# Attention and two expert stages on one core: the second expert's weights loaded after routing, tile stores moved to SP, q and k fetched two pairs ahead, first value means by matmul

## The chip, the cores and the metric

The kernel runs on one core of a Trainium2 chip (trn2). The metric is the device time of one execution in microseconds (us), lower is better. The inputs are float32 and the output is float32.

## What is computed

```python
# attention: B=2, H=8, S=768, D=64, block 32, window 16
k_sum = k.reshape(B, H, nb, block, D).max(axis=3)
v_sum = v.reshape(B, H, nb, block, D).mean(axis=3)
scores_l = scale * q @ k.T          # kept where |i-j| < 16, else -1e9
scores_s = scale * q @ k_sum.T + log(block)
a = softmax(concat(scores_l, scores_s))
x = a @ concat(v, v_sum)            # 1536 tokens of 512

# first expert stage: N=1536, 8 experts, D=512, F=1024, top 2
noisy = x @ w_gate + log1p(exp(x @ w_noise)) * noise
for e in range(E):                  # each token goes to its top two experts
    out[mask] += top2_w * (relu(x[mask] @ w1[e]) @ w2[e])

# second stage, dense: F=2048
h = x @ w_in; g = maximum(0.01 * h, h); out = g @ w_out
```

Every product with weights is made of three products of split numbers: a float32 is split into a part `hi` that TensorE takes in one pass and the rest `lo`, and hi·hi, lo·hi and hi·lo are added up in PSUM.

## The kernel before, in words

Each engine has its program in its own order, written out by hand; semaphores are all that ties them.

**Attention.** The 16 heads go in 8 pairs (`PAIRS`), a pair's 12 units of 64 rows in 3 groups (`GROUPS`), so there are 24 steps c. Per pair PE turns q (`turn_q`, L1044) and k (`turn_k`, L1053) by transposes, and per step it makes the scores (`score`, L1066), turns the probabilities (`turn_probs`, L1075) and weighs the values (`weigh`, L1090). Between them lie DVE's maximum and normalisation and ACT's exp and copies. PE's program for pair n is score(3n), turn_probs, turn_k(n+1), weigh, score(3n+1), ..., score(3n+2), turn_probs, turn_q(n+2), weigh(3n). Tokens of finished pairs are also turned and multiplied with the gate weights (L1103, L1112).

SP issues the loads and stores of this stage, in one queue: q and k of a pair (`load_q`, `load_k`), the windows of v for a pair (`load_windows`, three DMAs), the block means of v spread over the units (`load_means`), and the finished tokens (`store_x`). Rows of q, k and v are 256 bytes long and lie apart in the target, so a pair costs 2·2·768 = 3072 packets for q and k, 24·64 + 2·16·23 = 2272 for the windows, 2·24·12 = 576 for the means and 768 for the tokens, 6688 in all. There is one buffer `qk_nat` for q and k: q of pair n+1 is fetched once q of pair n has been turned. The block means come from POOL: `block_means(i)` (L465) halves 128 blocks of 32 rows six times, SP stores the result in HBM and reads it back; there are three such parts, and the first pair needs the first of them.

POOL then splits the weights of expert 0 and, from the fifth turned k on, of expert 1 (`load_weights`): 8 chunks of 512 KB, each a DMA (L476), `w_hi` (L495) and `w_lo` (L497), 4 staging buffers. `w1_ready` is raised after chunk 4, `w2_ready` after chunk 8. The split weights have two places (`par` 0 and 1), so expert e takes the place of e-2.

**Routing.** DVE, ACT and PE pick each token's experts, ending with `token_of` (L925), the token of every row of every tile. There are 31 tiles of 128 rows.

**First expert stage.** POOL gathers the tokens of each tile by indirect DMA: tiles 0 to 2 into `x_first` (L548), tiles 3 and up into a ring of 7 places `x_ring` (L538), from which POOL stores them tile by tile in HBM (`store_tile`, L529, 4 tiles behind the gather). A place is gathered into again once its store has landed. Tiles 3 to 23 are gathered in one go before the weights of expert 2, tiles 24 and 25 after them, 26 to 30 after those of expert 3.

SP reads a tile back into one of two places `x_row` (`load_row`, L373) and stores the tile's result from the single buffer `y_row` (`store_row`, L377): load_row(3), load_row(4), store_row(0), the filling of spare rows (L392), load_row(5), store_row(1), and so on. PE's program for tile t (`tile`, from L1223) is: turn x of t (L1177), second product of tile t-2 (hT and w2), turn h of t-1 (L1182), first product of t (L1190 for both products). Before the second product of t-2 PE waits here:

```python
                pe.wait_ge(w2_ready, loads)
                pe.wait_ge(hT_lo_ready, t + 1)
                if not first:
                    pe.wait_ge(y_ready, t)
```

and DVE does, per tile t of its loop, `xT_out(t)`, `y_out(t - 2)`, `hT_out(t - 1)`, where y_out copies the product out of PSUM:

```python
                if not first:
                    dve.wait_ge(y_stored, 16 * t)
                nc.vector.tensor_copy(y_row[:], bank).then_inc(y_ready, 1)
```

**Second stage.** Rows are picked by indirect DMA and PE makes the two dense products (L1274 to L1276, L1289 to L1291). The change doesn't touch it.

## Time and profile before

| | us |
|---|---|
| three runs | 831.04, 832.78, 834.69 |
| median | 832.78 |
| the profiled execution, its own time | 829.91 |
| its span | 828.3 |
| PE busy | 754.7 (91%) |
| POOL busy | 392.5 (47%) |
| DVE busy | 272.5 (33%) |
| ACT busy | 224.1 (27%) |

The span is the time from the first to the last instruction of the trace; the execution's own time is 1.6 us longer. By stages, in us from the span's start: attention until 130, routing until 153, the first expert stage until 545, the second to the end. Times below are positions in this one execution. "PE L1044 <- DMA qk_nat" in a table of waits reads: PE stood idle before the instruction of line 1044, and the DMA into qk_nat was what ended the wait.

### The profile page before, as it was taken

How to read it: one execution, taken by the hardware profiler on the slowest of the kernel's cores; microseconds unless marked ns; L12 is line 12 of the kernel's file. 1: busy time of each engine (PE TensorE's matmuls, PEld its weight loads, DVE VectorE, ACT ScalarE, POOL GpSimd, SP SyncE). 2: the span in 40 equal slices, each digit the busy share in tenths (PEclk: the TensorE clock that was granted, in tenths of full speed). 3: DMA queues.
4: the chain of work that ended last, by engine and by line, in shares of the span. 5: the costliest groups of instructions: out<-in, count | busy, mean ns of one | idle time of the engine just before them, and what ended most of it. 6: DMA issues, size and time to landing. Idle time of an engine off the chain costs nothing.

```text
span 828.3 us, 12304 instructions
## 1 busy us (share of the span) xinstructions
PE 754.7 (91%) x4026; PEld 632.2 (76%) x4027; DVE 272.5 (33%) x521; ACT 224.1 (27%) x405; POOL 392.5 (47%) x350
## 2 busy tenths in 40 slices
PE   3569892699999999999999999979999999999997
PEld 3458782578878888888888888878788887888885
DVE  3456556321221221222222122136343324432223
ACT  2557562022112212112112121225222222222221
POOL 5687860465786967888788783610011001000000
PEclk9889895599999999999999999989999999999999
DMA  9799970389726364353444441334011101010001
GB/s 213 177 286 227 268 128 13 112 288 297 242 89 215 127 214 173 120 187 143 144 142 156 138 141 38 114 127 154 13 39 51 51 1 50 0 51 0 0 1 51
DMA packets 87422, 103.15 MB, mean 125 GB/s; under 512 B 55680, under 2 KB 61824, under 8 KB 86976
## 3 DMA queue, kind: packets, MB, share of 16 engines
q0 software_dynamic: 17008, 59.52, 22.0%
q1 hardware_dynamic: 69328, 43.22, 20.5%
q8 instruction: 17, 0.28, 0.2%
q10 hardware_dynamic: 1056, 0.03, 0.1%
q14 instruction: 13, 0.11, 0.0%
HBM read 80.89 MB, written 23.69 MB: 126 GB/s over the span
## 4 chain that ended last, share of the span: by engine, by line
PE 61%; POOL 13%; DMA 10%; SPq 7%; DVE 4%; issue 4%; ACT 1%; POOLq 0%; DVEq 0%
PE p L1190 23%; POOL w_lo L497 6%; PE p L1274 5%; PE p L1276 5%; PE p L1275 5%; PE p L1289 5%; PE p L1291 5%; PE p L1290 5%; DMA x_by_tile<-x_ring 3%; POOL w_hi L495 3%; SPq L294 2%; DMA x_ring<-x_tokens,token_of 2%; POOL x_ring L538 2%; PE p L1182 2%; DMA stage<-in_moe_w 2%
## 5 line engine op out<-in xcount | busy, mean ns | idle before, releaser
L497 POOL TENSOR_TENSOR w_lo<-stage,w_hi 128x1024 fp32r<-128x1024 f32 x72 | 171.8, 2386 | 6.0
L1190 PE MATMUL p<-w_hi,xT_hi 128*128 x248 | 100.1, 404 | 3.3 <-DVE xT_lo L929 1.6
L584 POOL DMA_INDIRECT y_pick<-y_by_tile,slots x20 | 19.1, 955 | 165.9 <-PE p L1261 150.2
L1190 PE MATMUL p<-w_lo,xT_hi 128*128 x248 | 97.2, 392 | 0.0
L1190 PE MATMUL p<-w_hi,xT_lo 128*128 x248 | 97.2, 392 | 0.0
L1190 PE MATMUL p<-w_hi,hT_hi 128*128 x240 | 96.5, 402 | 0.0
L1190 PE MATMUL p<-w_lo,hT_hi 128*128 x240 | 93.9, 391 | 0.0
L1190 PE MATMUL p<-w_hi,hT_lo 128*128 x240 | 93.5, 390 | 0.0
L495 POOL TENSOR_SCALAR w_hi<-stage 128x1024 fp32r<-128x1024 f32 x72 | 75.9, 1054 | 18.9 <-DMA stage<-in_moe_w 14.8
L1274 PE MATMUL p<-f_xT_hi,w_hi 128*128 (+2 forms) x200 | 78.3, 392 | 1.3 <-DVE f_xT_lo L978 1.3
L1275 PE MATMUL p<-f_xT_lo,w_hi 128*128 (+2 forms) x200 | 77.2, 386 | 0.0
L1276 PE MATMUL p<-f_xT_hi,w_lo 128*128 (+2 forms) x200 | 77.1, 386 | 0.0
L1289 PE MATMUL p<-w_hi,f_hT_hi 128*128 128x512 f32 x192 | 75.0, 390 | 1.4 <-DVE f_hT_lo L988 1.3
L1291 PE MATMUL p<-w_hi,f_hT_lo 128*128 128x512 f32 x192 | 74.7, 389 | 0.0
L1290 PE MATMUL p<-w_lo,f_hT_hi 128*128 128x512 f32 x192 | 74.7, 389 | 0.0
L686 ACT CAST hT_hi<-p 128x1024 fp32r<-128x1024 f32 x30 | 30.5, 1015 | 156.5 <-PE p L1182 143.3
L929 DVE TENSOR_TENSOR xT_lo<-p,xT_hi 128x512 fp32r<-128x512 f32 x31 | 21.4, 692 | 154.6 <-ACT xT_hi L683 149.9
L986 DVE SCALAR_TENSOR_TENSOR f_h<-p,f_h 128x512 f32<-128x512 f32 x48 | 33.2, 691 | 116.6 <-ACT f_h L708 116.6
L681 ACT ACTIVATE h_row<-p 128x1024 f32<-128x1024 f32 x30 | 30.8, 1027 | 139.7 <-PE p L1190 134.6
L708 ACT COPY f_h<-p 128x512 f32<-128x512 f32 x48 | 28.2, 588 | 142.2 <-PE p L1276 142.2
L935 DVE COPY y_row<-p 128x512 f32<-128x512 f32 x31 | 21.5, 693 | 115.6 <-PE p L1190 115.6
L476 POOL DMA_DIRECT2D stage<-in_moe_w x64 | 41.5, 650 | 33.0 <-POOL w_lo L497 22.5
(184 smaller groups left out, 1253.8 us busy)
## 6 DMA issues: line engine op xcount, KB each, us to landing
stage<-in_moe_w POOLq DMA_DIRECT2D x64, 512.0 KB, 4.9
y_by_tile<-y_row SPq DMA_DIRECT2D x31, 256.0 KB
x_by_tile<-x_ring POOLq DMA_DIRECT2D x28, 256.0 KB, 6.9
x_row<-x_by_tile SPq DMA_DIRECT2D x28, 256.0 KB
qk_nat<-in_q SPq DMA_DIRECT2D x16, 192.0 KB, 5.6
qk_nat<-in_k SPq DMA_DIRECT2D x16, 192.0 KB, 4.7
stage<-in_v SPq DMA_DIRECT2D x3, 1024.0 KB, 7.8
v_win<-in_v SPq DMA_DIRECT2D x8, 384.0 KB
```

The costliest lines, as they stand in the source:

```text
L476: pool.dma_start(stage_view(c % STAGES, c), source(c)).then_inc(staged[c % STAGES], 16)
L495: pool.tensor_scalar(w_hi[:, par, cols], stage[:, c % STAGES, :], 1.0, 1.0, ALU.mult, ALU.mult).then_inc(hi_split, 1)
L497: pool.tensor_tensor(w_lo[:, par, cols], stage[:, c % STAGES, :], w_hi[:, par, cols].bitcast(F32), ALU.subtract).then_inc(lo_split, 1)
L681: nc.scalar.activation(h_row[:], h_bank[:], ACT.Relu).then_inc(h_ready, 1)
L986: nc.vector.scalar_tensor_tensor(out=h, in0=f_h_bank[c % 2], scalar=0.01, in1=h, op0=ALU.mult, op1=ALU.max).then_inc(f_leaky_done, 1)
L1190: last = nc.tensor.matmul(bank, a, w, start=(c == 0 and i == 0), stop=(c == left_hi.shape[1] - 1 and i == 2))
L1274: nc.tensor.matmul(to, hi, f_xT_hi[:, cols], start=(k == 0), stop=False)
L1275: nc.tensor.matmul(to, hi, f_xT_lo[:, cols], start=False, stop=False)
L1276: last = nc.tensor.matmul(to, lo, f_xT_hi[:, cols], start=False, stop=(k == KD - 1))
L1289: nc.tensor.matmul(f_y_bank[m], f_hT_hi[:, c % 2, rows], hi, start=(c == 0), stop=False)
L1290: nc.tensor.matmul(f_y_bank[m], f_hT_hi[:, c % 2, rows], lo, start=False, stop=False)
L1291: last = nc.tensor.matmul(f_y_bank[m], f_hT_lo[:, c % 2, rows], hi, start=False, stop=(c == FC - 1))
```

## The change

Six things move, and the line numbers of the changed kernel are up to 30 higher.

1. q and k have two buffers each (`qk_nat` and `qk_other`, which lies in the second place of w_hi) and are fetched up to two pairs ahead.
2. POOL loads expert 1 no longer during attention. Three of its chunks are fetched before `token_of`; the splitting stands after the gathers of tiles 3 to 9, and the gathers of tiles 10 to 23 stand between its chunks 4 and 5 (`between`).
3. `store_tile` goes from POOL to SP. SP's program is now: stores of tiles 3 to 9, load_row(3), load_row(4), stores of tiles 10 to 23, store_row(0), and from there as before.
4. The first pair's block means are made by PE: 12 small matmuls of the windows with `in_block` (1/32 where a row is in a block), one PSUM bank, one ACT copy. The three parts of `block_means` cover the other 14 heads, the last with 80 blocks, and are stored one by one inside SP's loop of pairs: each of the last two with a wait for its landing.
5. PE's first score comes before turn_q(1) and turn_k(1) comes later, with the same moves on ACT and DVE.
6. POOL builds `in_block` (four instructions) before the masks.

```diff
+MEAN_ROWS = [(2 * NB, 2 * NB + P), (2 * NB + P, 2 * NB + 2 * P), (2 * NB + 2 * P, B * H * NB)]
...
-LAG = 4
...
+        with ExitStack() as room:
+            sb("first_w_hi", [P, WCOLS], where=room)
+            qk_other = sb("qk_other", [P, 2, TPB, 2, D], where=room)
+            v_mean = sb("v_mean", [P, 3, D], where=room)
+            in_block = sb("in_block", [WK, 2 * NB - 2], where=room)
...
-            qk_nat = sb("qk_nat", [P, 2, TPB, 2, D], where=room)
+            qk_nat = [sb("qk_nat", [P, 2, TPB, 2, D], where=room), qk_other]
...
-            v_mean = xT_gate[:, 0:3 * D].rearrange("p (i d) -> p i d", i=3)
...
         def _(sp):
             def load_q(n):
                 for h in range(2):
-                    sp.dma_start(qk_nat[:, 0, :, h, :], q_pairs[2 * n + h]).then_inc(q_loaded, 16)
+                    sp.dma_start(qk_nat[n % 2][:, 0, :, h, :], q_pairs[2 * n + h]).then_inc(q_loaded[n % 2], 16)
...
             def load_rows(i):
 
-                sp.dma_start(stage[:, 2 * (i % 2):2 * (i % 2) + 2, :].rearrange("p a n -> p (a n)"),
-                             v_rows[i * P:(i + 1) * P, :]).then_inc(v_nat_loaded[i], 16)
+                first, end = MEAN_ROWS[i]
+                sp.dma_start(stage[0:end - first, 2 * (i % 2):2 * (i % 2) + 2, :].rearrange("p a n -> p (a n)"),
+                             v_rows[first:end, :]).then_inc(v_nat_loaded[i], 16)
...
@@ -320,42 +327,39 @@
 
             load_q(0)
             load_k(0)
-            load_rows(0)
             sp.wait_ge(consts_done, 2)
             load_windows(0)
+            load_q(1)
+            load_k(1)
+            load_rows(0)
+            load_windows(1)
             sp.wait_ge(q_turned, 1)
-            load_q(1)
+            load_q(2)
             sp.wait_ge(k_turned, 1)
-            load_k(1)
+            load_k(2)
+            store_means(0)
             load_rows(1)
-            sp.wait_ge(q_turned, 2)
-            load_q(2)
-            load_windows(1)
-            store_means(0)
-            load_rows(2)
             sp.wait_ge(v_mean_stored[0], 16)
-            load_means(0)
             load_means(1)
             for n in range(PAIRS):
-                if n + 2 < PAIRS:
+                if n + 3 < PAIRS:
+                    sp.wait_ge(q_turned, n + 2)
+                    load_q(n + 3)
                     sp.wait_ge(k_turned, n + 2)
-                    load_k(n + 2)
+                    load_k(n + 3)
+                if n == 0:
+                    load_rows(2)
                 if n >= 1:
                     store_x(n - 1, 0)
                     if n + 1 < PAIRS:
                         sp.wait_ge(weighed, GROUPS * n)
                         load_windows(n + 1)
+                        if n < 3:
+                            store_means(n)
+                            sp.wait_ge(v_mean_stored[n], 16)
                         load_means(n + 1)
                     store_x(n - 1, 1)
                     store_x(n - 1, 2)
-                if n + 3 < PAIRS:
-                    sp.wait_ge(q_turned, n + 3)
-                    load_q(n + 3)
-                if n == 0:
-                    for i in (1, 2):
-                        store_means(i)
-                    for i in (1, 2):
-                        sp.wait_ge(v_mean_stored[i], 16)
...
-            def load_row(t, r, uses):
-
-                sp.wait_ge(xs_stored[r], 16 * uses)
+            def load_row(t):
+
+                sp.wait_ge(xs_stored[(t - FIRST) % RING], 16 * ((t - FIRST) // RING + 1))
                 half = (t - FIRST) % ROWS
-                sp.dma_start(x_row[:, half, :], xs_dram[bass.ds(t * P, P), :]).then_inc(x_row_loaded[half], 16)
+                sp.dma_start(x_row[:, half, :], xs_dram[t * P:(t + 1) * P, :]).then_inc(x_row_loaded[half], 16)
 
             def store_row(t):
                 sp.wait_ge(y_ready, t + 1)
                 sp.dma_start(ys_dram[bass.ds(t * P, P), :], y_row[:]).then_inc(y_stored, 16)
 
-            def turn_over(t):
-
+            def store_tile(t):
                 r, uses = (t - FIRST) % RING, (t - FIRST) // RING + 1
-                if t >= FIRST + ROWS:
-                    sp.wait_ge(x_turned, t - ROWS + 1)
-                load_row(t, r, uses)
-                if t >= FIRST + 1:
-                    store_row(t - FIRST - 1)
-
-            assert (TILES - FIRST) % RING == 0
-            for t in range(FIRST, TILES):
-                turn_over(t)
-                if t == FIRST + 1:
+                sp.wait_ge(gathered[r], 16 * uses)
+                sp.dma_start(xs_dram[t * P:(t + 1) * P, :], x_ring[:, r, :]).then_inc(xs_stored[r], 16)
+
+            for t in range(FIRST, FIRST + RING):
+                store_tile(t)
+            for t in range(FIRST, FIRST + ROWS):
+                load_row(t)
+            for t in range(FIRST + RING, 2 * NT):
+                store_tile(t)
+            store_row(0)
+            for t in range(FIRST + ROWS, TILES):
+                if t >= 2 * NT:
+                    store_tile(t)
+                sp.wait_ge(x_turned, t - ROWS + 1)
+                load_row(t)
+                store_row(t - FIRST - 1)
+                if t == FIRST + ROWS:
                     sp.dma_start(ys_dram[FULL * P:TILES * P, :], x_dram[0:(TILES - FULL) * P, :]).then_inc(spare_filled, 16)
...
+
+            link(pool.memset(in_block[:], 0.0))
+            blocks = in_block[:, NB - 2:NB]
+            link(pool.memset(blocks, 1.0 / BLOCK))
+            link(pool.affine_select(out=blocks, in_=blocks, compare_op=ALU.is_ge, fill=0.0, base=-WINDOW, pattern=[[-BLOCK, 2]], channel_multiplier=1))
+            signal(pool.affine_select(out=blocks, in_=blocks, compare_op=ALU.is_ge, fill=0.0, base=WINDOW + BLOCK - 1, pattern=[[BLOCK, 2]], channel_multiplier=-1))
...
+            def fetch(source, c):
+                pool.dma_start(stage_view(c % STAGES, c), source(c)).then_inc(staged[c % STAGES], 16)
+
+            def load_weights(source, e, par, reused=True, fetched=False, between=None):
+
+                for c in range(0 if fetched else STAGES - 1):
+                    fetch(source, c)
...
+                    if c == KD and between:
+                        between()
...
             load_weights(lambda c: weight_piece(0, c), 0, 0, reused=False)
-            pool.wait_ge(k_turned, 5)
-            load_weights(lambda c: weight_piece(1, c), 1, 1, reused=False)
...
+            for c in range(STAGES - 1):
+                fetch(lambda c: weight_piece(1, c), c)
             pool.wait_ge(token_of_done, 1)
...
-            def store_tile(t):
-                r, uses = ring_slot(t)
-                pool.wait_ge(gathered[r], 16 * uses)
-                pool.dma_start(xs_dram[t * P:(t + 1) * P, :], x_ring[:, r, :]).then_inc(xs_stored[r], 16)
...
                         pool.wait_ge(xs_stored[r], 16 * (uses - 1))
                     pool.indirect_dma_start(out=x_ring[:, r, :], out_offset=None, in_=x_dram,
                                             in_offset=bass.IndirectOffsetOnAxis(ap=token_of[:, t:t + 1], axis=0)).then_inc(gathered[r], 16)
-                    if t - LAG >= first:
-                        store_tile(t - LAG)
-                for t in range(max(first, end - LAG), end):
-                    store_tile(t)
...
-            gather_tiles(FIRST, 2 * NT)
+            gather_tiles(FIRST, FIRST + RING)
+            load_weights(lambda c: weight_piece(1, c), 1, 1, reused=False, fetched=True, between=lambda: gather_tiles(FIRST + RING, 2 * NT))
...
-            q_part(1)
             for n in range(PAIRS):
                 c = GROUPS * n
                 if c >= 1:
                     probs_out(c - 1)
                 softmax_exp(c)
-                if n + 1 < PAIRS:
+                if n == 0:
+                    act.wait_ge(first_means_done, 1)
+                    nc.scalar.copy(v_win[WK:KC, 0, :, :, 0:D], first_mean_bank.rearrange("x (h d) -> x h d", h=2).unsqueeze(2).to_broadcast([NB, 2, UNITS, D])).then_inc(first_means_ready, 1)
+                    q_part(1)
+                elif n + 1 < PAIRS:
                     k_part(n + 1)
 
                 probs_out(c)
                 softmax_exp(c + 1)
+                if n == 0:
+                    k_part(1)
                 if n >= 2:
-                    if n == 2:
-                        for i in range(3):
-                            act.wait_ge(v_mean_stored[i], 16)
...
-            q_part(1)
-            dve.wait_ge(consts_done, 3)
+            dve.wait_ge(consts_done, 4)
             for n in range(PAIRS):
                 for g in range(GROUPS):
                     c = GROUPS * n + g
                     if c >= 3:
                         normalise(c - 3)
                     softmax_max(c)
-                    if g == 1 and n + 1 < PAIRS:
+                    if c == 0:
+                        q_part(1)
+                    if c == 2:
+                        k_blocks(1)
+                    if g == 1 and 1 <= n < PAIRS - 1:
                         k_blocks(n + 1)
                     if g == 2 and n + 2 < PAIRS:
...
-                if g == 0:
-                    pe.wait_ge(v_loaded[n % 2], 80 * (n // 2 + 1))
+                if c == 0:
+                    pe.wait_ge(first_means_ready, 1)
+                if g == 0 and n >= 1:
+                    pe.wait_ge(v_loaded[n % 2], (80 if n % 2 else 48) + 80 * (n // 2))
...
+            def first_means():
+
+                pe.wait_ge(v_loaded[0], 48)
+                pe.wait_ge(consts_done, 3)
+                for u in range(UNITS):
+                    last = nc.tensor.matmul(first_mean_bank, in_block[:, NB - 2 - 2 * u:2 * NB - 2 - 2 * u], v_win[0:WK, 0, :, u, 0:D],
+                                            start=(u == 0), stop=(u == UNITS - 1))
+                last.then_inc(first_means_done, 1)
...
-            turn_q(1)
             for n in range(PAIRS):
                 c = GROUPS * n
                 score(c)
                 if c >= 1:
                     turn_probs(c - 1)
-                if n + 1 < PAIRS:
+                if n == 0:
+                    first_means()
+                    turn_q(1)
+                elif n + 1 < PAIRS:
                     turn_k(n + 1)
                 if c >= 2:
                     weigh(c - 2)
 
                 score(c + 1)
                 turn_probs(c)
+                if n == 0:
+                    turn_k(1)
                 if n >= 2:
                     gate_turn(n - 2)
```

SP around the first expert stage; x_by_tile is the tiles' place in HBM, y_by_tile the results'. Before:

```order
L318 DMA x_tokens<-x_out 128x2x128 x3
L373 DMA x_row<-x_by_tile 128x512 x2
L377 DMA y_by_tile<-y_row 128x512
L392 DMA y_by_tile<-x_tokens 32x14336
L373 DMA x_row<-x_by_tile 128x512
L377 DMA y_by_tile<-y_row 128x512
```

and in the change:

```order
L325 DMA x_tokens<-x_out 128x2x128 x3
L386 DMA x_by_tile<-x_ring 128x512 x7
L377 DMA x_row<-x_by_tile 128x512 x2
L386 DMA x_by_tile<-x_ring 128x512 x14
L381 DMA y_by_tile<-y_row 128x512
L377 DMA x_row<-x_by_tile 128x512
L381 DMA y_by_tile<-y_row 128x512
L402 DMA y_by_tile<-x_tokens 32x14336
```

Twenty-one stores of tiles now stand in SP's program, fourteen of them ahead of the first store of a result.

POOL after routing, before:

```order
L548 DMA x_first<-x_tokens,token_of 128x512 x3
L538 DMA x_ring<-x_tokens,token_of 128x512 x5
L529 DMA x_by_tile<-x_ring 128x512
L538 DMA x_ring<-x_tokens,token_of 128x512
...
L529 DMA x_by_tile<-x_ring 128x512 x5
L476 DMA stage<-in_moe_w 128x1024 x3
```

and in the change:

```order
L557 DMA x_first<-x_tokens,token_of 128x512 x3
L553 DMA x_ring<-x_tokens,token_of 128x512 x7
L491 DMA stage<-in_moe_w 128x1024
L515 TENSOR_SCALAR w_hi<-stage 128x1024
L517 TENSOR_TENSOR w_lo<-stage,w_hi 128x1024
...
L491 DMA stage<-in_moe_w 128x2x512
L553 DMA x_ring<-x_tokens,token_of 128x512 x14
L515 TENSOR_SCALAR w_hi<-stage 128x1024
L517 TENSOR_TENSOR w_lo<-stage,w_hi 128x1024
```

The gathers of tiles 10 to 23 (x14) have four chunks of weights ahead of them and the other four behind.

SP in attention in the change, the second pair's turn of the loop:

```order
L286 DMA qk_nat<-in_q 128x6x64 x2
L290 DMA qk_nat<-in_k 128x6x64 x2
L325 DMA x_tokens<-x_out 128x2x128
L298 DMA v_win<-in_v 64x24x64
L299 DMA v_win<-in_v 16x23x64
L300 DMA v_win<-in_v 16x23x64
L318 DMA v_means<-v_mean 128x64
L307 DMA v_win<-v_means 24x12x64 x2
L325 DMA x_tokens<-x_out 128x2x128 x2
```

q and k stand at its head, for three pairs on, and the store of a part of the means stands with its wait between the windows and the reading of the means.

## Rows read from the trace of the kernel before

**Rows 1.** Windows: start:end length, busy us PE, PEld, DVE, ACT, POOL, PEclk, DMA share, GB/s
```profile
36.00:40.00 4.00, 4.00 (x54) 3.52 (x53) 2.85 (x7) 3.42 (x7) 3.13 (x7) 0.98 0.25 42
76.00:104.00 28.00, 22.96 (x225) 20.42 (x224) 15.83 (x36) 17.04 (x41) 21.50 (x18) 0.88 1.18 273
300.00:400.00 100.00, 99.65 (x487) 82.85 (x486) 21.57 (x25) 20.49 (x25) 78.30 (x63) 1.00 0.49 172
```
**Rows 2.** Waits of PE from 40 to 116: us in total, times, longest
```profile
PE p L1044 <- DMA qk_nat<-in_q: 9.6, 3, 5.4
PE p L1053 <- DMA qk_nat<-in_k: 3.0, 2, 2.1
```
**Rows 3.** Waits from 0 to 40
```profile
PE p L1090 <- DMA v_win<-v_means: 6.3, 1, 6.3
```
**Rows 4.** DMA queues from 76 to 104 (q1 SP's, q0 POOL's): packets, MB, share
```profile
q1 hardware_dynamic: 12839, 3.59, 74.9%
q0 software_dynamic: 1091, 4.01, 42.4%
```
**Rows 5.** DMA queues from 111 to 116
```profile
q1 hardware_dynamic: 2560, 0.81, 123.0%
```
**Rows 6.** Timeline of PE in attention: start, us, what [idle before, releaser]
```profile
33.54 2.06 PE L1066 MATMUL p<-kT,q_diag 128*128 128x120 f32 x8
...
58.58 1.54 PE L1044 MATMUL p<-ident,qk_nat 128*128 128x128 f32 x6 [5.44 <-DMA qk_nat<-in_q]
...
71.12 0.88 PE L1044 MATMUL p<-ident,qk_nat 128*128 128x128 f32 x6
```
**Rows 7.** Timeline of POOL: gathers of tiles 3, 4 and 23
```profile
157.00 0.95 POOL L538 DMA_INDIRECT x_ring<-x_tokens,token_of  x1 [0.30 <-issue]
158.25 0.94 POOL L538 DMA_INDIRECT x_ring<-x_tokens,token_of  x1 [0.30 <-issue]
...
200.77 0.97 POOL L538 DMA_INDIRECT x_ring<-x_tokens,token_of  x1 [0.30 <-DMA x_by_tile<-x_ring]
```
**Rows 8.** Timeline of POOL: chunk 1's w_hi and chunk 4's w_lo of expert 2
```profile
213.18 1.06 POOL L495 TENSOR_SCALAR w_hi<-stage 128x1024 fp32r<-128x1024 f32 x1 [2.05 <-DMA stage<-in_moe_w]
...
229.09 2.37 POOL L497 TENSOR_TENSOR w_lo<-stage,w_hi 128x1024 fp32r<-128x1024 f32 x1
```
**Rows 9.** Timeline of PE: first products of tiles 0 and 6, tile 2's second product
```profile
159.26 0.79 PE L1190 MATMUL p<-w_hi,xT_hi 128*128 x1 [1.60 <-DVE xT_lo L929]
...
162.69 0.40 PE L1190 MATMUL p<-w_lo,xT_hi 128*128 x1
...
199.48 0.48 PE L1190 MATMUL p<-w_hi,hT_hi 128*128 x1
...
231.74 0.49 PE L1190 MATMUL p<-w_hi,xT_hi 128*128 x1 [1.00 <-POOLq L500]
```
**Rows 10.** Timeline of DVE: tile 1's result, tile 2's hT_lo
```profile
193.09 0.69 DVE L935 COPY y_row<-p 128x512 f32<-128x512 f32 x1 [3.81 <-PE p L1190]
194.91 1.22 DVE L929 TENSOR_TENSOR hT_lo<-p,hT_hi 128x1024 fp32r<-128x1024 f32 x1 [1.13 <-ACT hT_hi L686]
```
**Rows 11.** Timeline of SP: store of tile 0's result
```profile
181.44 0.32 SPq L377 DMA_DIRECT2D y_by_tile<-y_row  x1
```
**Rows 12.** DMA queues from 157 to 208
```profile
q0 software_dynamic: 3306, 10.83, 66.6%
q1 hardware_dynamic: 976, 3.53, 19.7%
```
**Rows 13.** Issues over the whole span: out<-in, queue, count, KB each, median us to landing
```profile
out<-f_y SPq DMA_DIRECT2D x12, 256.0 KB, 2.0
...
x_ring<-x_tokens,token_of POOLq DMA_INDIRECT x28, 6.9
...
v_means<-xT_gate SPq DMA_DIRECT2D x3, 32.0 KB, 4.0
...
x_first<-x_tokens,token_of POOLq DMA_INDIRECT x3, 3.5
```

32 lines of the change are left out of this document (15 added, 17 removed).

## The prediction

> **What bounds the kernel now.** I read the busy table by stretches first, then PE's waits in attention, then the DMA queues, and last the order in time of POOL, PE and DVE after routing. In the first expert stage PE is the bound: 99.65 of 100 us [rows 1]. Whatever stops PE there is paid in full, and only what stands in POOL's or SP's programs ahead of something PE needs can stop it. In attention PE is busy 22.96 of 28 us in the stretch from 76 to 104, while the DMA share is 1.18 (packets overlap, so it passes 1) [rows 1]. PE stands idle for q 9.6 us and for k 3.0 us between 40 and 116 [rows 2], and 6.3 us for the first means [rows 3]. After the 5.4 us of idle before the turn of q at 58.58 that turn took 1.54 us, and the next, with none, 0.88 [rows 6]: so a stop also costs a stretch at half clock. Attention is thus set by transfers, and by those of SP's queue, on which q, k and v all lie.
>
> How fast is that queue? From 76 to 104, beside expert 1's weights, it moved 12839 packets in 28 us, 459 per us [rows 4]. From 111 to 116, with no weights beside it, 2560 in 5 us, 512 per us [rows 5]. The two rates are close although POOL's queue held 42.4% of the engines' time in the first and nothing in the second. The queue looks limited by its packets far more than by its neighbour. A pair has 6688 packets, 13.1 us at 512 per us; from one turn of q to the next (58.58 to 71.12) it was 12.5 us [rows 6].
>
> **The change in attention.** Taking expert 1's weights away: the 12839 packets would take 25.1 us at 512 per us in place of 28, a gain of **2.9**. The first pair's means are no longer fetched: 576 packets, **1.1**. From 36 to 40 the DMA share was only 0.25, since SP was waiting for means to land while q and k had one buffer [rows 1]; with q and k up to two pairs ahead there is work in the queue, 4 x 0.75 = **3.0**. The deeper fetch gives nothing beyond that as long as the queue itself is the bound: it can reorder 13.1 us of packets per pair, not shorten them. Sum: **7.0 us gained**. Bounds: two stores of means now stand in SP's loop with a wait for their landing, 4.0 us in the median [rows 13]; if each leaves the queue empty for 2.5 us, 7.0 - 5.0 = 2. Above, every wait of PE for a transfer goes: 9.6 + 3.0 + 6.3 = 18.9, and three stretches at half clock of 1.5 each, 23.4. I stay near the lower end because the two packet rates say so.
>
> The small edits I cost at nothing: the 12 matmuls and the copy for the first means fall where PE waited for means anyway [rows 3]; the four instructions for in_block come before masks that PE's first score doesn't use; expert 0's weights start later, with routing still ahead of their first use.
>
> **The change after routing.** Each time is in the clock of the trace before, with routing's end where it was.
>
> POOL: the gather of tile 3 starts at 157.00 and each takes 1.25 us with its gap [rows 7]. Seven without stores end at 165.7. One fetch later (some 0.8 us, an estimate) the splitting of expert 1 begins at 166.5. From chunk 1's w_hi to the end of chunk 4's w_lo it is 229.09 + 2.37 - 213.18 = 18.3 us [rows 8], so 184.8; another fetch and gap (1.6, estimate) and the gather of tile 10 starts at **186.4**. Before, all 21 gathers had been issued by 201.7. Now 14 stand after 186.4, and a ring place is only free once its store has landed.
>
> Their pace: at least 1.25 us each [rows 7]; at most what it was with stores, (200.77 - 157.00)/20 = 2.19 us [rows 7]. Between them: from 157 to 208 the engines moved 10.83 + 3.53 = 14.4 MB at 86.3% of their time [rows 12], so 0.33 MB per us when full, and a tile gathered and stored is 0.52 MB, 1.6 us. I take 1.6, since stores no longer queue behind later gathers and the filling of spare rows comes later. Tile 23's gather then starts at 186.4 + 13 x 1.6 = 207.2. It lands after 3.5 us quiet and 6.9 in a crowd [rows 13]; with 5, at 212.2.
>
> SP: store_row(0), issued at 181.44 before [rows 11], now stands behind the store of tile 23. Two issues of 0.3 us: 212.8. Its landing, 2.0 us for such a store in quiet and up to 4.0 beside others [rows 13], 2.5 taken: **215.3**. Who waits: DVE's y_out(1) needs the single y_row, done at 193.09 before, and behind it on DVE stands hT_out(2) [rows 10]. PE's second product of tile 2, at 199.48 before [rows 9], needs both. So 215.3 + 0.7 + 1.2 and 0.2 for the handings over = **217.4**, and PE stands 217.4 - 199.5 = **17.9 us**.
>
> After it PE starts at half clock. The first nine matmuls of tile 0 took from 159.26 to 162.69, the first 0.79 us and the ninth 0.40 [rows 9]; I charge 1.5 us. What is late next? Expert 1's w2, needed one tile later, comes after the last gather: 208.2 + 14 = 222, in the shadow of this wait (PE asks for it near 231). Expert 2's w1 came at 231.5, 23.1 us after POOL's last tile store; now 222 + 23 = 245, and PE asks at 230.7 + 19.4 = 250. So PE's wait of 1.0 us for it [rows 9] goes. Later experts have more room. **Loss: 17.9 + 1.5 - 1.0 = 18.4 us.** Bounds: pace 1.25, landings 3.5 and 2.0: PE starts at 210.9, loss 11.9. Pace 2.19, landings 6.9 and 4.0: 228.5, loss 29.5.
>
> **Sum.** 18.4 - 7.0 = +11.4 us. The profiled execution took 829.9, so 841.3 for such an execution; it lies 2.9 below the median of the three runs, and the same difference on the median, 832.8, gives **844**.
>
> **Rivals.** *Engines shared in attention.* If the two queues share the engines' time, q1 inherits what q0 held: 42.4% of 28 us, 11.9 us, at a share of 1.18 worth 10.1 in place of 2.9 [rows 1, 4]. Gain 14.2, net +4.2, **837**. For it: the share stands above 1 with both. Against it: 459 and 512 packets per us. The Trainium skill (DMA: Bandwidth & Descriptors, Queues, rings and completion order) says that each DMA engine goes round the queues that have work, a packet at a time; by that rule the freed turns are SP's and this rival holds. Rows 4 and 5 agree with it only in part, a rate 12% higher where it would ask for far more.
>
> *The ring stays slow.* Gathers at 2.19 us as before, because a store beside gathers lands as late as it did: 13 x 0.59 = 7.7 more, net +19, **852**. For it: DMA was 86% busy [rows 12]. Against it: part of that was the filling of spare rows and the single queue.
>
> *All DMA waits go.* The fetch two pairs ahead takes every wait for q, k and means off PE: gain 23.4, net -5.0, **828**, faster. It decides where SP's queue carries a pair's 6688 packets in the time that PE alone needs, some 10 us, so 650 per us and more. Nothing near that is in rows 4 or 5.
>
> *The second expert isn't hidden.* Should store_row(0) somehow not wait, PE would still come to expert 1's w2 near 212 and get it at 222: 10 us lost, net about +3, **836**. SP's program in the change speaks against its first half.
>
> The Trainium skill (DMA: Bandwidth & Descriptors, Specifications) gives about 358 GB/s as the share of HBM per core; by it a tile's 0.52 MB would take 1.46 us and not 1.6, an estimate that would bring the whole down by 1.8 us. No run here shows that limit by itself.
>
> **Chances.** The forecast (stop of 14 to 22 us, small gain in attention) 0.55; ring slow 0.15; engines shared 0.17; all waits gone 0.06; second expert alone 0.07. A measurement of this kernel tells a change from none beyond about 0.5%, 4.2 us. Faster takes the third rival and a corner of the second: 0.07. Within: the rest of the second and most of the last, 0.18. Slower: 0.75. The range leaves out the third rival and the far end of the slow ring: 832 to 856.
>
> **What would show it.** In the changed profile PE should stand idle once for 14 to 22 us before tile 2's second product, hT_lo on DVE ending that wait; SP should issue store_row(0) right behind the store of tile 23, near 213 less what attention gained; the last gather should be issued some 50 us after the first. Attention and routing should end about 7 us earlier, with 500 packets per us on SP's queue while no weights move. If the last gather comes within 45 us or attention ends 14 us earlier, the size is wrong; if PE does not stop at tile 4's start, the mechanism is.

## The result and the profile after

| | before | after |
|---|---|---|
| median of 8 runs each | 832.28 | 838.93 |
| lowest to highest | 828.73 to 835.3 | 837.49 to 843.19 |
| the profiled execution, its own time | 829.91 | 837.6 |
| its span | 828.3 | 836.0 |
| first gather on POOL | 153.09 | 143.19 |
| own time less first gather | 676.8 | 694.4 |

The ratio is 1.0085, its 95% interval 1.0055 to 1.0114: slower by a little under 1%, and inside the predicted range (832 to 856), 5 us below its centre. The last two lines cut the time of the profiled execution at the first gather, the point where attention and routing hand over to the experts. The part ahead of it became 9.9 us shorter, the part behind it 17.6 us longer. That cut is used below for all kernels but `e1_only`. Each rests on one profile per kernel, and the part ahead of the gather scatters by up to 6 us from profile to profile (see the table of all kernels).

First PE's waits of the changed kernel over the whole span: us in total, times, longest.

```profile
PE p L1220 <- DVE hT_lo L944: 15.9, 1, 15.9
PE p L1107 <- DMA v_win<-v_means: 12.2, 4, 6.8
PE p L1187 <- DVE r_sc L881: 9.6, 1, 9.6
PE p L1195 <- DVE at_row L914: 5.6, 1, 5.6
PE p L1059 <- DMA qk_nat<-in_q: 5.0, 1, 5.0
```

There is one stop of 15.9 us on hT_lo. The waits for q and k inside attention [rows 2] are gone: the 5.0 us left are those of the start. In their place stand four waits for the means, 12.2 us, where before there was one of 6.3 [rows 3].

The stop is read from three timelines. SP first, then DVE, then PE (start, length, what, and in brackets the idle time before it and what ended it):

```profile
180.28 21.40 SPq L386 DMA_DIRECT2D x_by_tile<-x_ring  x14
201.72 0.43 SPq L381 DMA_DIRECT2D y_by_tile<-y_row  x1
202.27 0.38 SPq L377 DMA_DIRECT2D x_row<-x_by_tile  x1
```

```profile
204.64 0.69 DVE L950 COPY y_row<-p 128x512 f32<-128x512 f32 x1 [24.28 <-DMA y_by_tile<-y_row]
205.25 1.21 DVE L944 TENSOR_TENSOR hT_lo<-p,hT_hi 128x1024 fp32r<-128x1024 f32 x1
```

```profile
190.21 0.60 PE L1207 MATMUL p<-ident,x_row 128*128 128x128 f32 x4
206.68 0.79 PE L1220 MATMUL p<-w_hi,hT_hi 128*128 x1 [15.88 <-DVE hT_lo L944]
207.27 0.63 PE L1220 MATMUL p<-w_hi,hT_lo 128*128 x1
...
212.39 0.59 PE L1220 MATMUL p<-w_hi,hT_lo 128*128 x1
212.81 0.40 PE L1220 MATMUL p<-w_lo,hT_hi 128*128 x1
213.05 0.40 PE L1220 MATMUL p<-w_hi,hT_hi 128*128 x1
```

SP works off fourteen tile stores in one block of 21.40 us, and the store of tile 0's result is issued right behind it at 201.72. DVE stands 24.28 us for that store's landing, ahead of the copy of tile 1's result, then makes hT_lo of tile 2, and PE starts. Until about 212.6 PE's matmuls follow each other at 0.43 us in place of 0.23, the lower of the two clocks: fourteen steps, some 2.8 us.

What held SP is seen on POOL's timeline: the first ring gather, the first behind expert 1's chunks, the two that waited for a ring place, and the last:

```profile
147.09 0.95 POOL L553 DMA_INDIRECT x_ring<-x_tokens,token_of  x1 [0.30 <-issue]
...
176.22 1.03 POOL L553 DMA_INDIRECT x_ring<-x_tokens,token_of  x1 [0.30 <-issue]
...
188.21 0.94 POOL L553 DMA_INDIRECT x_ring<-x_tokens,token_of  x1 [2.18 <-DMA x_by_tile<-x_ring]
...
192.58 0.94 POOL L553 DMA_INDIRECT x_ring<-x_tokens,token_of  x1 [2.19 <-DMA x_by_tile<-x_ring]
...
196.33 0.95 POOL L553 DMA_INDIRECT x_ring<-x_tokens,token_of  x1 [0.30 <-issue]
```

Behind tile 10 come 13 gathers in 20.1 us, 1.55 each: between the 1.25 of a gather that waits for nothing and the 2.19 of before [rows 7]. The pace isn't even: eleven steps take 1.25 us, and the two that wait for a place take 3.1.

In attention I read SP's queue by stretches. Its rows after (packets, MB, share), from 3 to 23 us with nothing beside it, and from 44 to 66 with expert 0's weights on POOL's queue:

```profile
q1 hardware_dynamic: 13463, 4.39, 118.1%
```

```profile
q0 software_dynamic: 1008, 3.67, 51.8%
q1 hardware_dynamic: 7564, 2.09, 46.7%
```

That is 673 packets per us alone and 344 beside weights. The 344 are a mean of unlike parts. From 44 to 52 us the weights held most of the engines' time and SP's queue moved 196 packets per us; from 52 to 60 it moved 613; behind that SP stood still until 64.03 for the landing of a store of means. The rows from 44 to 52, then from 52 to 60:

```profile
q0 software_dynamic: 575, 2.10, 74.7%
q1 hardware_dynamic: 1567, 0.52, 25.0%
```

```profile
q1 hardware_dynamic: 4904, 1.29, 85.8%
q0 software_dynamic: 201, 0.75, 36.0%
```

The 459 and 512 on which the prediction rested [rows 4, 5] are neither of them the queue's limit: the first is a rate beside weights, the second that of 5 us at the end of attention (see the part on the prediction).

### The profile page after: what moved, and what is told of

It reads as the page before. It is cut to its first block, busy times and chain, and to the rows that moved or that the text cites. A ratio compares the mean times of both kernels' runs of the same rounds, so it can differ in the third digit from the quotient of the medians.

```text
span 836.0 us, 12354 instructions
## 1 busy us (share of the span) xinstructions
PE 759.6 (91%) x4050; PEld 634.4 (76%) x4051; DVE 272.6 (33%) x521; ACT 225.0 (27%) x406; POOL 377.2 (45%) x326
## 4 chain that ended last, share of the span: by engine, by line
PE 77%; DMA 6%; issue 5%; POOL 4%; SPq 3%; DVE 3%; ACT 1%; DVEq 0%; POOLq 0%
PE p L1220 37%; PE p L1304 5%; PE p L1306 5%; PE p L1305 5%; PE p L1319 5%; PE p L1321 5%; PE p L1320 5%; PE p L1212 3%; DMA v_win<-v_means 2%; DMA x_ring<-x_tokens,token_of 1%; POOL x_ring L553 1%; PE p L1207 1%; DMA v_means<-v_mean 1%; POOL w_lo L517 1%; PE p L1081 1%
## 5 line engine op out<-in xcount | busy, mean ns | idle before, releaser
L1220 PE MATMUL p<-w_hi,hT_hi 128*128 x240 | 97.8, 408 | 15.9 <-DVE hT_lo L944 15.9
L515 POOL TENSOR_SCALAR w_hi<-stage 128x1024 fp32r<-128x1024 f32 x72 | 75.9, 1055 | 18.4 <-DMA stage<-in_moe_w 15.6
L698 ACT CAST hT_hi<-p 128x1024 fp32r<-128x1024 f32 x30 | 30.4, 1015 | 179.7 <-PE p L1212 164.1
L1321 PE MATMUL p<-w_hi,f_hT_lo 128*128 128x512 f32 x192 | 74.7, 389 | 0.0
L1320 PE MATMUL p<-w_lo,f_hT_hi 128*128 128x512 f32 x192 | 74.7, 389 | 0.0
L1220 PEld LDWEIGHTS p<-w_hi,hT_hi 128*128 128x128 f32 x240 | 45.8, 191 | 24.8 <-issue 16.1
```

The lines of the kernel that those rows point to most:

```text
L515: pool.tensor_scalar(w_hi[:, par, cols], stage[:, c % STAGES, :], 1.0, 1.0, ALU.mult, ALU.mult).then_inc(hi_split, 1)
L698: nc.scalar.copy(hT_hi[:].rearrange("p c m -> p (c m)"), hT_bank[:]).then_inc(hT_hi_ready, 1)
L1220: last = nc.tensor.matmul(bank, a, w, start=(c == 0 and i == 0), stop=(c == left_hi.shape[1] - 1 and i == 2))
L1320: nc.tensor.matmul(f_y_bank[m], f_hT_hi[:, c % 2, rows], lo, start=False, stop=False)
L1321: last = nc.tensor.matmul(f_y_bank[m], f_hT_lo[:, c % 2, rows], hi, start=False, stop=(c == FC - 1))
```

## The experiments

### The store of tile 0's result ahead of the fourteen tile stores

```
                 load_row(t)
+            store_row(0)
             for t in range(FIRST + RING, 2 * NT):
                 store_tile(t)
-            store_row(0)
```

> The changed kernel with one line moved: SP stores tile 0's result ahead of the fourteen stores of tiles 10 to 23 instead of behind them. Theory (the single y_row held behind the tile stores stops PE): PE's wait of 15.9 us before tile 2's second product goes entirely. The next thing late is expert 1's w2, ready 67.9 us after the start of the first gather in the changed kernel, while PE asks for it at 58.7: a wait of about 9.2 us one tile later. Net 6.5 us faster than the changed kernel, about 832. Rival (PE is held by the gathers or by weights, not by SP's order): the wait stays at 14 to 16 us at the same place and the time at 839.

Measured: 836.22 us, ratio to before 1.0059 (1.0029 to 1.0088). PE's waits of this kind in this kernel, then the same on PE's timeline:

```profile
PE p L1220 <- POOLq L520: 8.4, 2, 5.7
PE p L1207 <- DMA x_row<-x_by_tile: 2.2, 1, 2.2
```

```profile
208.31 0.66 PE L1207 MATMUL p<-ident,x_row 128*128 128x128 f32 x4 [2.21 <-DMA x_row<-x_by_tile]
214.67 0.79 PE L1220 MATMUL p<-w_hi,hT_hi 128*128 x1 [5.70 <-POOLq L520]
...
238.71 0.49 PE L1220 MATMUL p<-w_hi,xT_hi 128*128 x1 [2.71 <-POOLq L520]
```

The wait on hT_lo is gone, so its mechanism is shown. But of a stop of 15.9 us the median gave back only 2.7, which the two intervals don't tell from nothing, and the part behind the first gather only 4.6 (694.4 to 689.8). 10.6 us of other waits stood right behind, for SP's row load, expert 1's w2 and expert 2's w1: the row load behind the fourteen stores, the weights behind the same fourteen gathers in the middle of expert 1's chunks. Most of the cost thus lies in that block on POOL, as the next two kernels test, and not in the one store.

### Expert 1 unbroken, the gathers spread behind later experts

Two kernels. In both the store of tile 0 is issued first, POOL loads expert 1 without a break, and SP stores tiles in small lots between the row loads. `spread` gathers tiles 10 to 19 behind expert 2's chunks and all of 20 to 30 behind expert 3's; `spread2` splits the second block, 20 to 25 behind expert 3 and 26 to 30 behind expert 4. The edit of `spread2` against the changed kernel; the lines that it takes out of SP's program, the fourteen stores in one go among them, are left out:

```
+TILE_STORES = {9: range(10, 13), 10: range(13, 20), 13: range(20, 24), 14: range(24, 26), 18: range(26, 31)}
...
             load_weights(lambda c: weight_piece(2, c), 2, 0)
-            gather_tiles(2 * NT, 2 * NT + 2)
+            gather_tiles(FIRST + RING, 20)
             load_weights(lambda c: weight_piece(3, c), 3, 1)
-            gather_tiles(2 * NT + 2, TILES)
-            with pool.Fori(2, E // 2) as j:
+            gather_tiles(20, 26)
+            load_weights(lambda c: weight_piece(4, c), 4, 0)
+            gather_tiles(26, TILES)
+            load_weights(lambda c: weight_piece(5, c), 5, 1)
+            with pool.Fori(3, E // 2) as j:
```

> The changed kernel with the work after routing in another order: POOL splits expert 1 without gathers in between, gathers tiles 10 to 19 after expert 2 and 20 to 30 after expert 3; SP keeps the order of load_row and store_row and stores tiles in small lots between them. Theory (only the order on SP and POOL cost the 17.6 us between the first gather and the end): w2 of expert 1 is ready at about 47 us after the first gather, w1 of expert 2 at 70 (asked for at 77.7), of expert 3 at 122 (126.8), of expert 4 at 174 (175.9), so no wait of PE over 2 us from routing to the last tile, and 836 - 17.6 - 1.4 = 817 to 818 in span, 821 in the median. Rival (the weights of expert 1 can't be hidden after routing whatever the order): a wait of 5 us or more for weights remains, and 826 or more.

Measured for `spread`: 835.86 us, 1.0037 (1.0003 to 1.0071), not the 821 that was expected. Behind the start of the expert stage one wait of PE over 2 us was left:

```profile
PE p L1219 <- POOLq L519: 7.5, 1, 7.5
```

It is the same effect once more, three experts later: eleven gathers in one block made expert 4's w1 late. The profiled execution took 831.74 us, 4 us less than the median; what the others lost isn't shown.

> As the kernel whose gathers stand behind experts 2 and 3, with the last five gathers moved behind expert 4, since there PE waited 7.5 us for expert 4's w1 at tile 14: eleven gathers behind expert 3 took 22 us where 17 were free. Theory: six gathers behind expert 3 take 8 to 10 us, w1 of expert 4 is ready 174 us after the first gather, asked for at 176; that wait goes and no other comes; 8 us less than that kernel, span 822 to 825 for a first gather at 147, median 826 to 828. Rival (POOL is over its budget from expert 1 on, and a wait turns up at a later expert): 4 us or more of waits for weights remain.

Measured for `spread2`: 822.26 us over four runs, 0.9866 (0.9799 to 0.9933), faster than the changed kernel and than the one before. One wait for weights was left, 2.2 us. Since four runs are few, it was run again without an edit:

> The kernel spread2 a second time, without any edit, for an interval that says whether it is faster than the kernel before: its first four timed runs gave 0.987 with an interval from 0.980 to 0.993. If that is its place, the ratio is 0.985 to 0.991 (819 to 825 us against 832), and the profile again shows no wait of PE above 3 us between 152 and 500 us. If the four runs were lucky ones, it comes out at 0.994 to 1.0.

Measured: 822.36 us over six runs, 0.986 (0.9825 to 0.9896). PE's waits in that profile from 152 to 500 us:

```profile
PE p L1209 <- DMA x_first<-x_tokens,token_of: 4.0, 1, 4.0
PE p L1222 <- DVE xT_lo L946: 1.9, 2, 1.6
PE p L1214 <- ACT h_row L695: 0.7, 1, 0.7
PE p L1222 <- POOLq L519: 0.6, 1, 0.6
```

Nothing over 1 us is left that is not the start of the stage. In this profile own time less first gather is 824.63 - 149.30 = 675.3 us, as before the change (676.8), with the changed attention ahead of it.

### Only the second expert's weights moved

The kernel before, with expert 1's load taken out of attention and put behind the gathers of tiles 3 to 9; no second buffer, and the tile stores stay on POOL.

```
             load_weights(lambda c: weight_piece(0, c), 0, 0, reused=False)
-            pool.wait_ge(k_turned, 5)
-            load_weights(lambda c: weight_piece(1, c), 1, 1, reused=False)
...
-            gather_tiles(FIRST, 2 * NT)
+            gather_tiles(FIRST, FIRST + RING)
+            load_weights(lambda c: weight_piece(1, c), 1, 1, reused=False)
+            gather_tiles(FIRST + RING, 2 * NT)
```

> The kernel before with one thing changed in attention: expert 1's weights are loaded after the gathers of tiles 3 to 9 instead of during attention. Only the start of the first gather is read, 153.1 in the kernel before. Theory of the prediction (SP's queue is limited by its packets, hardly by its neighbour): 2.9 us earlier, 150. Rival (the engines are shared): 10.1 us earlier, 143, or as much as PE's waits for q and k after 76 allow, some 7. The total gets longer by PE's wait for expert 1, which isn't what is asked.

Measured: one run, 862.91 us; the first gather at 147.70, 5.4 us earlier than before. SP's queue from 76 to 96 us, where expert 1's weights used to be, and PE's longest waits:

```profile
q1 hardware_dynamic: 13346, 3.72, 107.7%
```

```profile
PE p L1190 <- POOLq L500: 35.9, 3, 32.3
PE p L1044 <- DMA qk_nat<-in_q: 19.8, 4, 8.7
```

That is 667 packets per us. The row of the kernel before from 80 to 100 us, with the weights in flight, gives 454:

```profile
q1 hardware_dynamic: 9079, 2.49, 69.9%
```

So weights on the other queue take a third of SP's rate. The share of the engines' time by the packets moved says how: 24.6 ns of an engine for each of SP's packets beside the weights, 25.8 without them (share times 16 engines times 20 us, by the packets; an estimate). A packet of SP's costs no more beside weights; there are fewer of them.

The 5.4 us are one profile's, no more than the scatter ahead of the gather. The freed stretch by itself says more: from PE's scores of pair 4 to those of pair 7 it took 38.3 us before (72.59 to 110.93) and 30.4 here (74.10 to 104.47), 8.0 less, where the prediction's theory asked for 2.9 and its rival for 10.1 or as much as PE's waits allow. All of the 19.8 us for q lie ahead of this stretch: from 74 us to the end of attention PE waited for no transfer at all. The 35.9 us say that behind routing this load needs the change's other parts (tile stores off POOL, first fetches early), which weren't tried one by one.

### The order of SP's program in attention

`means_early` issues the second and third store of means one pair ahead of their wait, so that SP doesn't stand for their landing. `windows_first` does that and also puts the loads of q and k for pair n + 3 behind the windows and means of pair n + 1.

```
+                if n == 1:
+                    store_means(1)
...
                         if n < 3:
-                            store_means(n)
                             sp.wait_ge(v_mean_stored[n], 16)
...
                     store_x(n - 1, 2)
+                if n == 1:
+                    store_means(2)
```

> The changed kernel with the second and third part of the means stored as soon as POOL has made them (ahead of pair 0's token stores, and at the end of the loop's second turn), so that SP does not stand still behind the windows. Theory (SP's two waits of 3.3 and 6.1 us empty its queue and end in PE's waits of 4.1 and 6.8 us): both waits of PE shrink to under 2 us together or move to q and k, attention ends 5 to 9 us earlier, routing's end at 134 to 138 instead of 143.2, and the time falls by as much, to 830 to 834. Rival (the queue's packets are the limit, 13.1 us a pair): PE's waits move to other transfers and the end of routing moves by under 2 us.

Measured: 835.43 us, 1.0035 (1.0008 to 1.0063). SP's two waits for these landings (3.3 and 6.1 us in the changed kernel) are gone, and PE waits for the means about as long as in the changed kernel (12.2 us there):

```profile
PE p L1110 <- DMA v_win<-v_means: 13.6, 3, 6.6
```

> The changed kernel with SP's loop in attention in another order: windows and means of the next pair first, q and k for three pairs on last (and the second and third part of the means stored as soon as they are made). Theory (in SP's one queue the 3072 packets of a q and k that PE needs two pairs later stand ahead of the windows and means that it needs next): PE's waits for means, 12.2 to 14.1 us in four profiles of this attention, fall to 5 or less and no wait for q or k over 3 us takes their place; the first gather starts at 138 to 140 instead of 143 to 147; time 3 to 6 us less than the changed kernel's. Rival (the packets up to that point are too many for the queue whatever their order): the same waits move to q and k, the first gather stays at 143 to 147.

Measured: 836.21 us, 1.0056 (1.0023 to 1.0089). PE's waits on transfers in this kernel, that of the start among them:

```profile
PE p L1062 <- DMA qk_nat<-in_q: 13.0, 2, 7.7
...
PE p L1062 <- DMA qk_other<-in_q: 2.7, 1, 2.7
```

The means' waits are gone, and q's are back at 15.7 us. The order decides which transfer is late, and by how much was not shown to change. Both medians are 2.7 to 3.5 us below the changed kernel's 838.93, with intervals that overlap; a gain of that size isn't shown.

### The fetch two pairs ahead taken back

```
-                if n + 3 < PAIRS:
-                    sp.wait_ge(q_turned, n + 2)
-                    load_q(n + 3)
-                    sp.wait_ge(k_turned, n + 2)
-                    load_k(n + 3)
+                if n >= 1 and n + 2 < PAIRS:
+                    sp.wait_ge(q_turned, n + 1)
+                    load_q(n + 2)
+                    sp.wait_ge(k_turned, n + 1)
+                    load_k(n + 2)
```

> The changed kernel with q and k fetched one pair ahead instead of two, two buffers kept. Theory (the second pair of lead only puts packets ahead of windows and means in the same queue): PE's waits for means shrink from 12 to 14 us to 5 to 8, those for q and k stay under 4, the time is the same as the changed kernel's or up to 4 us less. Rival (the lead is what gained in attention): waits for q and k of 8 us or more, first gather at 147 or later, and slower than the changed kernel.

Measured: 840.5 us, 1.0112 (1.0082 to 1.0143), beside 1.0085 (1.0055 to 1.0114) for the changed kernel: no difference that can be told. PE waited 17.5 us for q, the start among them, and not for means. The same edit on `spread2`, where no stop in the expert stage could cover it:

> spread2 with the edit of one_ahead: q and k are again fetched one pair ahead, with both buffers still there. In the changed kernel that edit gave 840.5 beside 838.9, within the interval, with waits for q of 17.5 us in place of waits for means of 12.2. If the fetch two pairs ahead is worth nothing because the total of the transfers decides, this stays within 2 us of spread2 (820 to 824). If the stall behind the routing had hidden its worth, as the gain of the other order in spread2_wf (817.3 beside 822.4) may suggest, it is 3 to 6 us slower (825 to 828), with the first gather near 150.

Measured: 820.19 us, 0.9869 (0.9828 to 0.991), beside 0.986 for `spread2`. The second pair of lead is worth nothing measurable; it turns waits for q into waits for means. Both kernels still have two buffers and fetch one pair ahead, so what the buffers are worth isn't tested by them.

### The first means through memory again

Rows 0 to 127 are again loaded (ahead of the first windows), added up, stored and read back, with no matmuls and no copy for them. The matmuls left out are twelve, not the 24 that the expectation names.

```
-MEAN_ROWS = [(2 * NB, 2 * NB + P), (2 * NB + P, 2 * NB + 2 * P), (2 * NB + 2 * P, B * H * NB)]
+MEAN_ROWS = [(0, P), (P, 2 * P), (2 * P, B * H * NB)]
...
             sp.wait_ge(v_mean_stored[0], 16)
+            load_means(0)
             load_means(1)
...
-                if n == 0:
-                    first_means()
-                    turn_q(1)
+                if n == 0:
+                    turn_q(1)
```

> The changed kernel with its fourth part alone undone: the value means of the first pair go again through the stored array (rows 0 to 127 loaded, added up on POOL, stored, read back six times for each head) instead of 24 matmuls on PE and a copy on ACT; everything else as changed. My step priced this part at 1.1 us of the gain, because only the 576 packets of the read mattered: then the time is 1 us above the changed kernel (about 838 against 836 to 839), with the first gather 1 us later. A rival says that the wait at the first weighing comes back whole (6.3 us in the kernel before, at 32.41) and pushes everything behind it, as the queue cannot catch up: then PE's first weighing moves from 25 us to about 32, and the time is 5 to 7 us above (842 to 846). A second rival says that the stretch from 44 to 80 us is held by the queue anyway and swallows it: 0 us, and the waits for the later means become shorter by what the first one costs.

Measured: 839.61 us, 1.0088 (1.0056 to 1.012). On PE's timeline the wait at the first weighing is back whole, and the later ones shrink:

```profile
31.58 1.19 PE L1104 MATMUL p<-v_win,probsT 120*64 120x65 f32 x16 [7.22 <-DMA v_win<-v_means]
...
54.55 0.74 PE L1104 MATMUL p<-v_win,probsT 120*64 120x65 f32 x16 [2.59 <-DMA v_win<-v_means]
...
69.25 1.19 PE L1104 MATMUL p<-v_win,probsT 120*64 120x65 f32 x16 [4.36 <-DMA v_win<-v_means]
```

The rival of 5 to 7 us falls. 1 us and 0 us can't be told apart by the time. Against the changed kernel's profile PE's scores of pair 1 start 6.8 us later, those of pair 4 2.6 and those of pair 5 0.8 (82.26 beside 81.45); that the delay is absorbed speaks for the queue's total as the limit, but these are single profiles.

### Expert 0's weights out of attention too

```
-            load_weights(lambda c: weight_piece(0, c), 0, 0, reused=False)
             pool.wait_ge(k_turned, PAIRS)
...
+            load_weights(lambda c: weight_piece(0, c), 0, 0, reused=False)
```

> The changed kernel with expert 0's weights also taken out of attention: POOL loads them once the last k is turned, ahead of routing's end. Theory (the engines are shared: SP's queue moved 344 packets per us beside the weights from 44 to 66 and 607 per us from 76 to 96 without): PE's waits for means fall from 12 to 14 us to under 6, attention ends 6 to 10 us earlier; expert 0 takes 38 us from about 90, done at 130, before or about when the first gather can start, 134 to 138. Time 830 to 833. Rival (SP's queue is limited by its own packets, as the prediction had it): under 3 us earlier, 836 or more.

Measured: 840.43 us over four runs, 1.0102 (1.0036 to 1.0168). SP's queue from 44 to 66 us, now alone:

```profile
q1 hardware_dynamic: 13266, 3.70, 86.8%
```

603 packets per us in place of 344. PE's scores of pair 4 start at 60.43 against 67.82 in the changed kernel, those of pair 5 at 71.20 against 81.45 and those of the last pair at 91.26 against 101.51; in the other profiles of the changed attention the last pair starts at 103 to 107. The first gather still came at 145.36, inside the 143 to 149 of those profiles. The ten microseconds were given back at the end of attention, where the weights now ran beside the last pair's means and the stores of the attention output:

```profile
104.87 1.19 PE L1105 MATMUL p<-v_win,probsT 120*64 120x65 f32 x16 [5.28 <-DMA v_win<-v_means]
```

Behind that wait PE had only the lower clock. Its granted clock from 104 to 122 us was 0.50 (the field behind POOL's), where the changed kernel had 0.99 from 108 to 121, and twelve gate products took 2.74 us in place of 1.51:

```profile
104.00:122.00 18.00, 15.45 (x100) 13.82 (x100) 2.78 (x13) 2.35 (x4) 16.83 (x12) 0.50 0.37 105
```

### Both together

> spread2 with the order of windows_first in the attention: the window values and the means of a pair are issued before the queries and keys of the pair three ahead, and the second and third store of the means are issued a pair earlier. In the changed kernel that order turned the waits for the means (12.2 us) into waits for q (15.7 us with that of the start), and the time stayed within 0.3%. If the queue's total between 44 and 80 us decides, this too stays within 2 us of spread2 (820 to 824). If the order matters once the stall behind the routing is gone, it falls by 3 to 5 us (817 to 819).

Measured: 817.29 us over six runs, 0.9826 (0.9792 to 0.9859), the best of the study, 14.5 us under the kernel before. Its interval overlaps `spread2`'s, so the gain by spreading the gathers is shown and a further 5 us by the order in attention is not.

### All kernels cut at the first gather

| kernel | own time | first gather | difference |
|---|---|---|---|
| before | 829.91 | 153.09 | 676.8 |
| after | 837.6 | 143.19 | 694.4 |
| means_early | 840.51 | 146.72 | 693.8 |
| windows_first | 836.77 | 142.38 | 694.4 |
| one_ahead | 840.59 | 146.77 | 693.8 |
| e0_late | 840.04 | 145.36 | 694.7 |
| row0_first | 836.22 | 146.38 | 689.8 |
| means_by_store | 838.73 | 145.49 | 693.2 |
| spread | 831.74 | 147.38 | 684.4 |
| spread2 | 825.98 | 145.35 | 680.6 |
| spread2_again | 824.63 | 149.30 | 675.3 |
| spread2_wf | 823.79 | 146.76 | 677.0 |
| spread2_one | 819.7 | 143.76 | 675.9 |

The changed kernel and its variants in attention alone agree behind the gather within 1.5 us, those of `spread2` within 1.7, but for its first profile, which had a wait of 2.2 us for weights and some 3 us more that I didn't follow. Ahead of it even one and the same attention program scatters: the changed one's first gather came at 143.19, 146.38 (`row0_first`), 147.38 (`spread`), 145.35 (`spread2`) and 149.30 (`spread2_again`). The scatter arises beside expert 0's weights: PE's scores of pair 2 start at 34.8 to 36.1 us in these five profiles, those of pair 4 at 67.7 to 74.6.

## Why the prediction was right

**The loss behind routing: 18.4 forecast, 17.6 measured.** The mechanism came as written: SP's store of tile 0's result behind the store of tile 23, DVE's single y_row, hT_lo of tile 2, PE. Counted from the first gather, that of tile 10 came 33.0 us later (33.3 forecast), the last one 53.1 (54.1 forecast), at a pace of 1.55 (1.6 forecast). SP's issue came at 201.72 where 212.8 less the 9.9 gained gives 202.9. DVE's copy came 2.9 us behind that issue (2.5 forecast), and PE's second product of tile 2 at 206.68, 17.1 us later behind the first gather than before (63.5 against 46.4), where I had 17.9. Of these 17.1, 15.9 are the stop; 1.0 PE had lost already in tile 0, which took longer at the lower clock and stands in no term of mine. The stretch at half clock was mis-sized: 1.5 forecast by the start of tile 0, some 2.8 measured. The term of -1.0 held: PE waits for no weights of expert 2, and with the other small wait for weights before it is 1.4. The pace of 1.6 came out as a mean, but not as the even pace of full engines from which it was worked out: it is eleven steps of 1.25 and two of 3.1. The terms as measured give 17.1 + 2.8 - 1.4 = 18.5, 0.9 above the 17.6 of the whole. Of that rest 0.6 lies in the second stage: from its first dense product to the end it was 280.7 us before and 280.1 after, and the lower clock at its start ended some 5.7 us behind that product before and some 3.6 after.

**What is late next** I had only for the case as changed. `row0_first` shows that the stop of 15.9 us covered 10.6 us of others. My last rival put the wait for w2 alone at 10 us and the result at 836; `row0_first` comes to 836.22, but by 5.7 us of w2, 2.7 of w1 and 2.2 of the row load, so that the number agrees is luck.

**The gain in attention: 7.0 forecast, 9.9 in the profiled execution.** The 9.9 are the largest of five: the changed attention's five first gathers lie at 146.3 in the mean, 6.8 us ahead of the kernel before, of which there is one profile. That the sum came near this is luck: the first of its three terms rests on a wrong reading, and the other two aren't borne out.

The failed step of the first is the sentence that the queue looks limited by its packets far more than by its neighbour, with 512 packets per us as its rate alone. The stretch from 111 to 116 had no weights, and it wasn't short of work: the engines' share was 1.23 [rows 5], and 1.42 from 111 to 114. But SP issued only means and stores of tokens in it, no q, k or windows. Its row from 111 to 114, 535 packets per us:

```profile
q1 hardware_dynamic: 1604, 0.41, 142.1%
```

Why these go at 535 and not at 667 wasn't followed; their rate doesn't hold for a whole pair. The runs show 673 alone at the start of attention, 667 and 603 in the stretches from which weights were taken, and 454 beside expert 1's. So the first rival had the mechanism: queues share the engines. It is also the rule of the Trainium skill (DMA: Bandwidth & Descriptors, Queues, rings and completion order) that engines go round the queues a packet at a time. The trace now agrees that the turns of an empty queue go to the other: 9079 packets in 20 us became 13346. The rival's own gain of 14.2 didn't come either. PE's scores show where the changed kernel was ahead: by 8.5 us at pair 2 (34.88 against 43.41), by 4.8 at pair 4 (67.82 against 72.59), by 9.4 at pair 7 (101.51 against 110.93). What the start gave was half taken back beside expert 0's weights, where PE waited 4.1 and 6.8 us for the means, and the freed stretch gave 4.6. Of the 8.5, 5.6 stood at the first score already (11.95 against 17.58): the new order at the start, which stands in none of my terms. No experiment took it out by itself.

The other two terms aren't borne out as single terms, either. The hole from 36 to 40 filled (DMA share 1.08 in place of 0.25), but it is filled in `one_ahead` too (1.15), and no run has a single buffer with the rest of the change; the 3.0 us are thus not tested. The first means' 576 packets were priced at 1.1, and the medians lie 0.7 apart, which can't be told from 0. What I didn't see is that expert 0's weights beside the packets of pairs 2 to 5 set the pace, so that an earlier start only reaches that stretch earlier; `e0_late` and `means_by_store` speak for it.

**The bound of 2** was named by the stores of means in SP's loop, each with a wait for landing. That wait exists, 3.3 and 6.1 us on SP, and `means_early` shows that taking it away moves the waits rather than removing them.

**The total**: -7.0 + 18.4 = 11.4 forecast, -9.9 + 17.6 = 7.7 in the profiled execution and 6.65 in the medians. The rest of 1 us between the two is less than the scatter of the attention part, and one profile doesn't show how that part scatters in the kernel before.

**All DMA waits go** fell: PE waited 12.2 us for means and 5.0 for q. Its condition, 650 packets per us, was met without weights only. **The ring stays slow** fell: 1.55 us per gather.

**Left open.** Whether expert 1's weights could stay in attention beside the spread gathers wasn't tried: the second buffer of q and k lies in the memory of the second w_hi, and both don't fit at once. What decides whether the same attention ends at 143 or 149 isn't settled, nor what the new order at the start is worth in time.

## What to carry to other kernels

Work that is moved behind a hand-over is paid there by what queues behind it on the same engine: before moving a block onto a queue, list every later instruction of that queue by its due time, and split the block until none is late; removing the first late one only uncovers the next (15.9 us of stop, 10.6 right behind it). A queue's rate read from a few us with the engines busy need not hold for another stretch (535 and 667 per us here), and a mean over a stretch in which the issuing engine stood still hides what happened (196, then 613 in a mean of 344); take the rate from a long stretch with the same mix of transfers and no holes. In the three reorderings tried here the waits changed their names, and no gain in time was shown.

## What the runs showed of the hardware

SP's queue, with most packets under 512 bytes, moved 603 to 673 packets per us when no weights were in flight. Beside packets of weights of some 3.6 KB that held 45.8% of the engines' time it moved 454, and each of its packets held an engine no longer than without them (24.6 and 25.8 ns, an estimate from shares and counts). Over 8 us in which the weights held 74.7%, it moved 196 per us. So a queue of few and large packets, 909 in 20 us, took a third of the rate of one with many small ones. A stop of 15.9 us was followed by some 2.8 us lost at the lower clock, more than the 1.5 us at the start of the expert stage before; and after a stop of 5.3 us in `e0_late` the granted clock was still at the lower level, 0.50 over the whole stretch from 104 to 122 us. And the same attention program, run in different kernels, reached its end up to 6 us apart, more than any single edit to it was shown to bring.
